# Weighing a whole attention head with the values stationary, in the slots of the next head

## The reference

```python
# q, k, v: (2, 8, 768, 64): 16 heads of 768 tokens by 64; proj: (64, 6)
q_bucket, k_bucket = ...            # 6 sign bits of q @ proj and k @ proj
mask = q_bucket[:, :, :, None] == k_bucket[:, :, None, :]
scores = np.where(mask, scale * (q @ k.T), -1e9)
attn = np.exp(scores - max(scores)); attn /= attn.sum() + 1e-9
attn_out = attn @ v                 # 768 x 64 for each head
x = attn_out as (1536, 512)         # then the experts, then the feed-forward layer
```

## Time and profile before

| | |
|---|---|
| median of 3 runs | 570.3 us (566.44 to 573.83) |
| the profiled execution | 567.69 us |
| its span, first to last instruction | 565.9 us |
| around the span | 1.8 us |
| PE busy | 506.3 us, 89% |
| DVE, ACT, POOL busy | 312.7, 303.1, 126.9 us |
| attention, first transposes of probabilities to the start of the second stage | 23.93 to 295.12 us |

### The profile page before, as it was taken

How to read it: one execution, slowest core, us unless ns; L and a number is a source line. 1 busy time by engine, 2 the same in 40 slices (tenths; PEclk the granted TensorE clock), 3 DMA queues, 4 the chain that set the end, 5 groups by cost and what they waited for, 6 DMA issues and landing times.

```text
span 565.9 us, 8762 instructions
## 1 busy us (share of the span) xinstructions
PE 506.3 (89%) x3378; PEld 411.0 (73%) x3378; DVE 312.7 (55%) x500; ACT 303.1 (54%) x449; POOL 126.9 (22%) x83
## 2 busy tenths in 40 slices
PE   4599999999999999999996776677698889998996
PEld 3489999999999999999993222123387668886874
DVE  4244555545555454555535311016999897888850
ACT  2367667676666767666655100002744775676650
POOL 3130303003030210300000000005333455454641
PEclk9999999999999999999999796789999999999999
DMA  8897373596645972371009499992000020001001
GB/s 195 183 189 165 68 171 64 111 344 146 151 85 129 329 159 67 76 199 67 1 10 395 190 379 393 377 378 107 1 2 0 0 75 0 1 0 74 0 0 74
DMA packets 49333, 75.76 MB, mean 134 GB/s; under 512 B 24752, under 2 KB 27696, under 8 KB 48688
## 3 DMA queue, kind: packets, MB, share of 16 engines
q1 hardware_dynamic: 48792, 73.85, 44.2%
q10 hardware_dynamic: 504, 1.39, 1.1%
HBM read 51.45 MB, written 3.15 MB: 96 GB/s over the span
## 4 chain that ended last, share of the span: by engine, by line
PE 76%; DMA 7%; DVE 7%; issue 3%; SPq 2%; ACT 2%; POOL 1%; DVEq 0%; POOLq 0%
PE o_acc L288 32%; PE unit L288 30%; PE unit L894 11%; DMA w<-in_moe_w 6%; DVE fu L795 2%; DVE g L806 1%; PE o_acc L860 1%; DVE fe L790 1%; SPq L325 1%; PE unit L950 1%; POOL g_lo L506 1%; ACT fe L612 1%; DMA turned<-in_q 1%; DMA vn<-in_v 1%; DVE fv L798 1%
## 5 line engine op out<-in xcount | busy, mean ns | idle before, releaser
L675 DVE TENSOR_REDUCE nmax<-unit 128x1 f32<-128x768 f32 x96 | 91.9, 957 | 123.5 <-PE unit L288 123.5
L541 ACT ACTIVATE probs<-unit,shift,keep 128x768 f32<-128x768 f32 x96 | 95.3, 993 | 94.1 <-DVE shift L678 94.1
L288 PEld LDWEIGHTS o_acc<-vn,turned 128*128 128x128 f32 x1152 | 136.5, 191 | 4.8 <-issue 0.5
L288 PE MATMUL o_acc<-vn,turned 128*128 128x64 f32 x1152 | 138.7, 270 | 0.3 <-DMA vn<-in_v 0.3
L288 PE MATMUL unit<-op 128*128 128x512 f32 (+1 forms) x384 | 93.1, 366 | 6.1 <-DMA op<-bit 6.1
L506 POOL TENSOR_TENSOR g_lo<-g,g_hi 128x1024 fp32r<-128x1024 f32 x24 | 73.0, 3040 | 88.3 <-ACT g_hi L619 88.3
L894 PE MATMUL unit<-ident,probs 128*128 128x128 f32 x576 | 80.6, 277 | 1.3 <-ACT probs L541 1.3
L549 ACT COPY turned<-unit 128x768 f32<-128x768 f32 x96 | 75.7, 788 | 1.3 <-PE unit L894 1.2
L288 PEld LDWEIGHTS unit<-op 128*128 128x128 f32 x384 | 60.2, 195 | 15.2 <-issue 10.8
L894 PEld LDWEIGHTS unit<-ident,probs 128*128 128x128 f32 x576 | 68.0, 152 | 1.9 <-issue 1.8
L288 PE MATMUL unit<-wo_hi,g_hi 128*128 128x512 f32 x96 | 38.9, 405 | 12.4 <-DVE m_pack L784 5.5
(11 more groups left out here) (120 smaller groups left out, 585.3 us busy)
## 6 DMA issues: line engine op xcount, KB each, us to landing
w<-in_moe_w SPq DMA_DIRECT2D x16, 2048.0 KB, 11.8
op<-cuts SPq DMA_DIRECT2D x31, 384.0 KB
op<-cuts SPq DMA_DIRECT2D x31, 192.0 KB
w_in_sb<-in_moe_w_in SPq DMA_DIRECT2D x1, 4096.0 KB, 19.6
wo_raw<-in_moe_w_out SPq DMA_DIRECT2D x2, 2048.0 KB, 17.0
vn<-in_v SPq DMA_DIRECT2D x8, 384.0 KB, 3.4
out_x<-stage SPq DMA_DIRECT2D x12, 256.0 KB, 2.4
qn<-in_q SPq DMA_DIRECT2D x14, 192.0 KB, 4.3
```

What stands on the lines that cost most here:

```text
L288: return nc.tensor.matmul(out_, lhsT, rhs, start=start, stop=stop, skip_group_check=True)
L541: sc.activation(probs[i % 3][:, :], unit("S", i)[:, 0:S], ACT.Exp, bias=shift[:, g % 4, t:t + 1], scale=keep[:, g % 4, t:t + 1], accum_out ...
L675: ve.tensor_reduce(nm, unit("S", i)[:, 0:S], AX.X, ALU.max, negate=True).then_inc(max_done, 1)
```

## The change

The weighing is turned round and moved. Per key tile k of head g the values (128x64) now stand in the array, and the turned probabilities of all six query tiles (128x768) stream past in two halves of 384 columns: half e = 0 goes to the column group that writes output partitions 0 to 63, half e = 1 to that of partitions 64 to 127. `weigh(g, k)` is these two products; six k sum one head. They run in the slots of head g + 1: in each second slot (s = 1, 3, 5), behind the scores, two key tiles in a row.

The result is now feature by query in one bank. ScalarE copies it (`copy_out`, 128x384, at the head of slot (g + 2, 0), ahead of `copy_probs`), TensorE transposes it back by three 128x128 transposes (`turn_out`, side piece "F" in slot (g + 2, 1)), and VectorE's `norm(g)` follows in that slot instead of slot (g + 1, 0). After the last slot come turn_out(14), the whole weighing of head 15 and turn_out(15).

For this `turned` becomes two tiles of 128x6x768 (one per head) instead of three of 128x6x128. That room is found by laying the second buffers of q and k where expert weights go later. From pair 2 on, all q and k loads share one place: `load_qk(n + 1)` now waits for the last transposes of pair n, before for those of pair n - 1. The side pieces use the bank of head h. `load_w1(2)` waits for the last spreads.

```diff
@@ -57,8 +57,11 @@
...
         pair = h // 2 + 1 if h % 2 == 0 else (h + 3) // 2
+        if s == 1 and h >= 2:
+            return "F", h - 2
         if pair >= NP or s < 2:
...
@@ -109,23 +112,29 @@
...
         att_at = top[0]
-        qn = [sb(f"qn{n}", [P, T, 2, D]) for n in range(2)]
-        kn = [sb(f"kn{n}", [P, T, 2, D]) for n in range(2)]
+        W1, SLOT = 4 * C * F, 4 * (C * F + FC * DM)
+        ring_at = (nc.sbuf_usable_end - 2 * SLOT) // 32 * 32
+        early_at = [ring_at]
+        rows_const = sb("rows_const", [P, 4, S], at=early_at)
+        qn = [sb(f"qn{n}", [P, T, 2, D], at=early_at if n else None) for n in range(2)]
+        kn = [sb(f"kn{n}", [P, T, 2, D], at=early_at if n else None) for n in range(2)]
         qk_t = sb("qk_t", [P, 2, S])
+        cuts = sb("cuts", [P, 4, S], F32R)
...
         op = [sb(f"op{n}", [P, 4, S], F32R, at=e_at if n < 2 else None) for n in range(PLACES)]
-        cuts = sb("cuts", [P, 4, S], F32R)
         bit = sb("bit", [P, HS], F32R)
...
-        turned = [sb(f"turned{n}", [P, T, P]) for n in range(3)]
-        first_qk = [t[:, :, :].rearrange("p k q -> p (k q)").rearrange("p (h t d) -> p h t d", h=2, t=T)
-                    for t in turned[0:2]]
+        turned = [sb(f"turned{n}", [P, T, S]) for n in range(2)]
+        first_qk = [t[:, 0, :].rearrange("p (h t d) -> p h t d", h=2, t=T) for t in turned]
+        ot = sb("ot", [P, HS])
         hash_w = sb("hash_w", [P, 32])
...
@@ -134,10 +143,6 @@
...
-        W1, SLOT = 4 * C * F, 4 * (C * F + FC * DM)
-        ring_at = (nc.sbuf_usable_end - 2 * SLOT) // 32 * 32
-        rows_const = sb("rows_const", [P, 4, S], at=[ring_at])
         assert e_at[0] <= att_at
...
@@ -203,9 +208,9 @@
...
         (t_done, t_copied, hi_done, lo_done, hashed, bits_done, bits_scaled, keys_done, max_done, shifted, exp_done,
-         p_turned, p_by_act, pv_done, den_done, rden_done, normed) = sems(
+         p_turned, p_by_act, pv_done, o_copied, o_turned, den_done, rden_done, normed) = sems(
             "t_done t_copied hi_done lo_done hashed bits_done bits_scaled keys_done max_done shifted exp_done "
-            "p_turned p_by_act pv_done den_done rden_done normed")
+            "p_turned p_by_act pv_done o_copied o_turned den_done rden_done normed")
         w_in_in, wo_in = sem("w_in_in"), sems("wo_in0 wo_in1")
...
@@ -253,7 +258,14 @@
...
         def rest_bank(h):
-            return o_bank(h + 1)
+            return o_bank(h)
+        def qk_place(n):
+            return 1 if n == 1 else 0
+        def qk_loads(n):
+            return 1 if n == 1 else n - 1
...
@@ -334,16 +346,16 @@
...
             def load_qk(n):
-                b = n % 2
+                b = qk_place(n)
                 if n >= 2:
-                    sp.wait_ge(t_done, t_pieces(n - 2, 1))
+                    sp.wait_ge(t_done, t_pieces(n - 1 if n > 2 else 0, 1))
                 for h in range(2):
...
                 if n >= 2:
-                    sp.wait_ge(pv_done, 6 * (2 * (n - 2) + 2))
+                    sp.wait_ge(pv_done, 2 * (n - 2) + 2)
                 sp.dma_start(vn[n % 2][:, :, :, :], v_h[:, 2 * n:2 * n + 2, :, :]).then_inc(v_in[n % 2], 16)
...
@@ -397,6 +409,9 @@
...
+            for g in (G - 2, G - 1):
+                done, count = ops_of(g)
+                sp.wait_ge(done, count)
             load_w1(2)
...
@@ -543,10 +558,19 @@
...
+                g, t = i // T, i % T
                 act.wait_ge(p_turned, i + 1)
-                if i >= 3:
-                    act.wait_ge(pv_done, i - 2)
-                sc.copy(turned[i % 3][:, :, :].rearrange("p k q -> p (k q)"), unit("P", i)[:, 0:S]).then_inc(p_by_act, 1)
+                if g >= 2:
+                    act.wait_ge(pv_done, g - 1)
+                sc.copy(turned[g % 2][:, :, t * P:(t + 1) * P], unit("P", i)[:, 0:S].rearrange("p (k q) -> p k q", q=P)
+                        ).then_inc(p_by_act, 1)
+            def copy_out(g):
+                act.wait_ge(pv_done, g + 1)
+                if g >= 1:
+                    act.wait_ge(o_turned, g)
+                sc.copy(ot[:, :], o_bank(g)[:, 0:HS]).then_inc(o_copied, 1)
...
@@ -564,12 +588,16 @@
...
                 i = T * h + s
+                if s == 0 and h >= 2:
+                    copy_out(h - 2)
                 copy_probs(i)
...
                     exponentials(i + LEAD)
+            copy_out(G - 2)
+            copy_out(G - 1)
...
@@ -685,10 +713,12 @@
...
                 ve.reciprocal(rden[:, :], den[:, :]).then_inc(rden_done, 1)
-                dve.wait_ge(pv_done, T * (g + 1))
+                dve.wait_ge(o_turned, g + 1)
                 dve.wait_ge(rden_done, g + 1)
-                ve.tensor_tensor(x_cols(g), o_bank(g)[:, 0:T * D].rearrange("p (t d) -> p t d", t=T),
-                                 rden[:, :].unsqueeze(2).broadcast_to([P, T, D]), ALU.mult).then_inc(normed, 1)
+                ve.tensor_tensor(x_cols(g).rearrange("p (e t) d -> p e t d", e=2),
+                                 o_bank(g)[:, 0:T * D].rearrange("p (t e d) -> p e t d", t=3, e=2),
+                                 rden[:, :].rearrange("p (e t) -> p e t", e=2).unsqueeze(3).broadcast_to([P, 2, 3, D]),
+                                 ALU.mult).then_inc(normed, 1)
...
@@ -705,10 +735,11 @@
...
                     bits(piece[1], rest_bank(h))
+                if piece and piece[0] == "F":
+                    norm(piece[1])
                 if T * h + s + LEAD < T * G:
                     row_max(T * h + s + LEAD)
-                if s == 0 and h > 0:
-                    norm(h - 1)
+            norm(G - 2)
             norm(G - 1)
...
@@ -840,8 +871,8 @@
...
                 else:
-                    pe.wait_ge(qk_in[n % 2], 64 * ((n + 1) // 2))
-                src = (qn, kn)[x][n % 2]
+                    pe.wait_ge(qk_in[qk_place(n)], 64 * qk_loads(n))
+                src = (qn, kn)[x][qk_place(n)]
                 for t in range(T):
...
@@ -851,11 +882,12 @@
...
                 if part == 0:
-                    pe.wait_ge(normed, h)
-                    pe.wait_ge(qk_in[n % 2], 64 * ((n + 1) // 2))
+                    if h >= 2:
+                        pe.wait_ge(normed, h - 1)
+                    pe.wait_ge(qk_in[qk_place(n)], 64 * qk_loads(n))
                 else:
                     pe.wait_ge(t_copied, i)
-                src = (qn, kn)[part // 2][n % 2]
+                src = (qn, kn)[part // 2][qk_place(n)]
                 for t in range(3):
...
@@ -894,24 +926,33 @@
...
-            def weigh(i):
-                g, t = i // T, i % T
-                pe.wait_ge(p_by_act, i + 1)
-                if t == 0 and g >= 2:
-                    pe.wait_ge(normed, g - 1)
-                for piece in [side_piece(g - 1, s) for s in range(T) if t == 0 and g >= 1]:
-                    if piece and piece[0] == "T":
-                        pe.wait_ge(t_copied, piece[1] + 1)
-                    if piece and piece[0] == "H":
-                        pe.wait_ge(bits_done, piece[1] + 1)
-                if t == 0 and g % 2 == 0:
-                    pe.wait_ge(v_in[g // 2 % 2], 16 * (g // 4 + 1))
-                for k in range(T):
-                    ins = mm(o_bank(g)[:, D * t:D * t + D], turned[i % 3][:, k, :], vn[g // 2 % 2][:, g % 2, k, :],
-                             k == 0, k == T - 1)
-                ins.then_inc(pv_done, 1)
+            def weigh(g, k):
+                if k == 0:
+                    pe.wait_ge(p_by_act, T * (g + 1))
+                    if g >= 2:
+                        pe.wait_ge(normed, g - 1)
+                    if g % 2 == 0:
+                        pe.wait_ge(v_in[g // 2 % 2], 16 * (g // 4 + 1))
+                    for piece in [side_piece(g, s) for s in range(T)]:
+                        if piece and piece[0] == "T":
+                            pe.wait_ge(t_copied, piece[1] + 1)
+                        if piece and piece[0] == "H":
+                            pe.wait_ge(bits_done, piece[1] + 1)
+                for e in range(2):
+                    ins = mm(o_bank(g)[D * e:D * e + D, 0:HS], vn[g // 2 % 2][:, g % 2, k, :],
+                             turned[g % 2][:, k, HS * e:HS * (e + 1)], k == 0, k == T - 1)
+                if k == T - 1:
+                    ins.then_inc(pv_done, 1)
+            def turn_out(g):
+                pe.wait_ge(o_copied, g + 1)
+                for t in range(3):
+                    f = slice(t * P, (t + 1) * P)
+                    ins = nc.tensor.transpose(o_bank(g)[:, f], ot[:, f], ident[:, :])
+                ins.then_inc(o_turned, 1)
...
@@ -930,14 +971,20 @@
...
                 if piece and piece[0] == "H":
-                    if h > 0:
-                        pe.wait_ge(normed, h)
+                    if h >= 2:
+                        pe.wait_ge(normed, h - 1)
                     hashes(piece[1], rest_bank(h))
+                if piece and piece[0] == "F":
+                    turn_out(piece[1])
```

(10 more changed lines are left out.)

## The result

| | before | after |
|---|---|---|
| median | 570.31 us (566.44 to 573.83, 4 runs) | 535.42 us (531.34 to 538.40, 4 runs) |
| ratio | | 0.940, 95% interval 0.933 to 0.947 |
| span of the profiled execution | 565.9 us | 536.6 us |
| second stage starts (first transposes of x) | 295.12 us | 261.77 us |
| from there to the end | 270.8 us | 274.8 us |

The change makes the kernel 34.9 us faster by the medians, 6%. The forecast was 535. In the profiled execution attention ends 33.35 us earlier; 33.5 were forecast.

A forecast was written before the change was run, and what follows sets the result against it. TensorE's work was taken to bound attention, with the softmax loop nearly closed. Later heads -34.7, head 0 -3.8, tail +5.0 sum to -33.5 us; span 565.9 becomes 532.4, with 1.8 around it 534.2, forecast 535 us, range 522 to 549.

The forecast's parts named there:

- W: Weighing of two key tiles in attention: 1.61 us, as 1.29 for four rounds plus 0.32 for the split.
- The 0.32 for going in and out: Cost in us of entering and leaving the column-group split, read from the hash products' slot, paid three times a head.
- The upper bound, 1.92: Weighing of two key tiles if each two rounds pay the split cost: 1.92 us, total 547 us; rival, chance 0.12.
- The column groups: Weighing: two groups of 64 run together; the rival, one after the other, gave 598 us, chance 0.05.
- The loop: Scores, row maximum, exponentials, transposes, next scores: 4.09 us for two slots, adding only 0.02 to TensorE's 4.35.
- Rival 4: Softmax in attention: hand-overs between three engines 0.3 us dearer a pair of slots, total 548 us; chance 0.08.
- "T" pairs: Pairs of attention slots that also hold turn_half transposes as side work: 5.14 us a pair.
- turn_out, copy_out, norm: First pair of slots of a head: turn_out adds 0.33 us, making 4.70; copy_out and norm cost nothing.
- Head 0: First head of attention, now without weighing: 3.8 us saved.
- Tail: End of attention, from the last slot's transposes to the second stage: 11.0 us, before 6.05; costs 5.0.
- Queues: SP's queue: the q and k load takes about 3 us, spreads start 3 to 8 us later, at no cost.
- The second stage: Everything after attention: 270.8 us before and after; a moved length would be a sign of being wrong.

The follow-up runs named there:

- the short maximum: The changed kernel with the row maximum taken over 128 of the 768 scores (softmax wrong where a maximum is missed): 525.92 us, ratio 0.924 to the kernel before.

## Why the prediction was right

- **TensorE was the bound.** Of the 37.4 us of busy time that left TensorE in attention, 33.35 left attention.
- **W.** Forecast 1.61. Measured 1.44 from start to start, 0.09 more in the step of the scores in front (0.88 for 0.79, in the run with the short maximum, where no loop interferes) and 0.05 in the step behind: 1.58. I had looked for 1.6 from start to start; a part of it shows in the neighbours. Single passes start in pairs, 0.007 us apart, in steps of 0.32, as forecast. The 0.32 for going in and out, taken from "H", was right to 0.03. The upper bound, 1.92, did not hold, nor did the estimate of 1.94 by the packing ratio of the Trainium skill, "TensorE: Matmul & The Clock Gate", Measured speedup vs the span model. The drain that the Trainium skill, "TensorEngine Tiling (Array Packing)", Key Properties, speaks of agrees with the 0.29 of a switch there and back in the run with one key tile a slot.
- **The column groups.** Inferred from groups of 32 and 4, shown for 64: passes in pairs, and 2.72 us with one group. What would have decided against the change, W = 2.3, is passed by that run, at 2.85 with both ends.
- **The loop.** The mis-sized term. Plain pairs 4.45 instead of 4.37: TensorE's own steps 4.30 instead of 4.35, the loop 0.15 instead of 0.02. Over attention the loop cost 8.2 us (the short maximum), of which 2.7 in head 0 and 0.5 in the last slot; so 5 us in the other pairs, where the forecast had about 2. It didn't show in the total: each head is out by at most 0.24, some up, some down, TensorE's own steps were 0.05 a pair shorter and the tail 0.4 shorter than forecast. That attention was hit to 0.2 us is luck of that kind. Rival 4 had the mechanism, at 0.3 a pair twice too dear.
- **"T" pairs.** 5.20 and 4.96, mean 5.08, forecast 5.14.
- **turn_out, copy_out, norm.** Pairs of slots with `turn_out` took 4.70 by forecast. They take 4.68 in odd heads and in even ones more: head 8 took 14.63, so its first pair 14.63 - 5.30 - 4.45 = 4.88. There `copy_out` meets a ScalarE that comes late out of the "T" slots. "Cost nothing" was wrong for `copy_out` by 0.2 in half of the heads, and for `norm` in the heads without side pieces: moving it took 0.28 off heads 13 and 14.
- **Head 0.** 3.73 us shorter (18.32 to 14.59), forecast 3.8. **Tail.** 4.54 longer, forecast 5.0.
- **Queues.** No wait for operands behind the first. The queue of SP after, around the load of q and k for the last pair:

```profile
155.70 4.20 SPq L337 DMA_DIRECT2D op<-bit  x4
...
168.71 0.64 SPq L353 DMA_DIRECT2D qn<-in_q  x1
...
176.00 0.67 SPq L311 DMA_DIRECT2D op<-cuts  x1
...
179.98 5.00 SPq L337 DMA_DIRECT2D op<-bit  x4
```

  The bits of head 11 are out at 159.90. The load of q and k goes at 168.71, held by the last "T" of head 9, and takes till 175.90, with 4 MB of weights on the way; the spread of head 12 starts behind it, at 176.00. Forecast were 3 us for the load and a start 3 to 8 us late; the load took 7.2, and in the kernel before the same one takes 14.9, from 182.26 to 197.18. Nothing waits for it.
- **The second stage.** I took 270.8 us before and after. In the twelve profiles since it was 270.2 to 275.0. Windows of the second stage, before and after:

```profile
295.12:565.90 270.78, 226.10 (x1106) 147.76 (x1106) 164.55 (x150) 118.06 (x131) 80.97 (x28) 0.94 0.34 128
```

```profile
261.77:536.60 274.83, 230.18 (x1106) 149.79 (x1106) 164.42 (x150) 118.05 (x131) 82.20 (x28) 0.92 0.33 126
```

  The same instructions, at a granted clock of 0.94 and 0.92: the 8 passes that took 3.70 us at 384.77 take 5.40 at 352.33 here. The two executions of the change had 274.8 and 273.8. Of the ten others, the six whose attention ends before 262 us had 270.5 to 275.0, the four in which it ends later 270.2 to 270.7. So it moves from execution to execution, and by these few profiles more often where attention is short; whether an earlier end changes its odds was not tested, and the runs of the kernel before lie at least as far apart (566.4 to 573.8 us). The second stage's length had been named as a sign of being wrong, and in the profiled execution of the change, 538.4 us, it moved by 4.0 us; attention there is as forecast. That the median came out at 535.4 against 535 rests in part on how these 4 us fall.

## What to carry to other kernels

A pass with a narrow moving side (64 columns) took 1.28 / 12 = 0.107 us, where at the rate of the 384-column passes it would be 0.054; how much of the rest is the load of its weights was not measured. Turned round, with two column groups side by side, the weighing cost 3 x 1.58 = 4.7 us a head instead of 7.7 (and 0.33 to turn the result back), and without the second group 3 x 2.85 = 8.6. The 0.29 us for going into the split and back is paid by the burst, so gather bursts; but count the latency that each burst covers: a burst for each two tiles kept a latency of 3.5 us nearly hidden, one for each three left it bare and lost 27 us. When a price is read in one slot, ask in which other slots its cover is the same before multiplying.

## What was unexpected of the hardware

- Going from two column groups of 64 straight to four of 32 costs about half of going in and out: the hash products took 0.78 us instead of 0.96 alone, 0.14 above their rounds instead of 0.32.
- The cost of the switch lies in four places: 0.09 us in the step of the products in front, 0.05 behind the first pair of passes (0.373 us to the second pair, later pairs 0.322), 0.10 behind the last pair (0.42 to the transposes), 0.05 in the step of the transposes. The weighing's own step, 1.44, hides a tenth of its price.
